# The first batch of a fused attention, mixing and gating kernel: other load queues, other owners for three steps, and four output buffers

## The reference

```python
def _attn_ref(q, k, v):
    B, H, S, D = q.shape
    factor = 4
    ...
    q_d = q.reshape(B, H, Sd, factor, D).mean(axis=3)
    ...
    out_d = sm_attn(q_d, k_d, v_d)
    out_up = np.repeat(out_d, factor, axis=2)
    pos = np.arange(S)
    mask = np.abs(pos[:, None] - pos[None, :]) < factor
    scores = scale * np.matmul(q, k.transpose(0, 1, 3, 2))
    scores = np.where(mask, scores, -1000000000.0)
    ...
    out_local = np.matmul(attn, v)
    return (out_up + out_local).astype(np.float32)

def _moe_ref(x, w_ch1, w_ch2):
    X = np.fft.fft(x, axis=1)
    X = np.fft.fft(X, axis=2)
    mixed = np.real(X).astype(np.float32)
    u = x + mixed
    ...
    un = (u - mu) / np.sqrt(var + 1e-06)
    ch = np.maximum(un @ w_ch1, 0.0) @ w_ch2
    return (u + ch).astype(np.float32)

def _moe2_ref(x, w_val, conv_w, w_out):
    ...
    gate = 1.0 / (1.0 + np.exp(-gate_pre))
    val = x @ w_val
    return (gate * val @ w_out).astype(np.float32)
```

## Time and profile before

| | |
|---|---|
| median of 3 runs | 759.3 us (758.93 to 759.83) |
| the profiled execution | 760.19 us, of which its span 758.3 us |
| TensorE matmul busy | 696.6 us, 92% of the span |
| VectorE, ScalarE, GpSimd busy | 393.0, 186.2, 168.8 us |
| chain that ended last | TensorE 79%, DMA 7%, VectorE 4%, GpSimd 3%, SP's queue 3% |

### The profile page before, as it was taken

The page is one execution under the profiler, slowest core; times in us unless marked ns, Lnnn a source line. Parts: engine busy times, 40 slices in busy tenths (PEclk is TensorE's granted clock), DMA queues, the critical chain, the costliest instruction groups (busy, mean ns, idle before and its releaser), DMA issues.

```text
span 758.3 us, 14783 instructions
## 1 busy us (share of the span) xinstructions
PE 696.6 (92%) x5936; PEld 531.9 (70%) x5936; DVE 393.0 (52%) x937; ACT 186.2 (25%) x405; POOL 168.8 (22%) x155
## 2 busy tenths in 40 slices
PE   2559857999999998999999999999999999999998
PEld 1445445877777776877777877877767877777776
DVE  4437585554644881544845871545754841123451
ACT  1536532222212132322112122221112131111101
POOL 8001477992101221003101321022201200000000
PEclk9999767999999999999999999999999999999999
DMA  9995047213001128025100027034100000000001
GB/s 254 280 243 154 5 169 170 50 50 74 18 2 32 32 63 204 16 57 114 34 1 32 32 69 204 10 78 100 27 1 1 17 24 24 1 1 2 1 24 39
DMA packets 47174, 51.35 MB, mean 68 GB/s; under 512 B 9149, under 2 KB 40192, under 8 KB 46022
## 3 DMA queue, kind: packets, MB, share of 16 engines
q1 hardware_dynamic: 32608, 31.06, 16.4%
q10 hardware_dynamic: 9574, 16.99, 7.2%
q0 software_dynamic: 4928, 2.39, 1.7%
HBM read 43.32 MB, written 4.72 MB: 63 GB/s over the span
## 4 chain that ended last, share of the span: by engine, by line
PE 79%; DMA 7%; DVE 4%; POOL 3%; SPq 3%; issue 2%; ACT 1%; ACTq 0%; POOLq 0%; DVEq 0%
PE Y L597 23%; PE P L580 23%; PE Y L702 4%; PE P L713 4%; PE P L702 4%; DMA kl<-qk_win 3%; PE A L609 3%; PE Y L713 3%; PE A L663 2%; DMA out<-ot 2%; PE A L567 2%; PE A L549 2%; PE A L652 1%; SPq L449 1%; PE A L502 1%
## 5 line engine op out<-in xcount | busy, mean ns | idle before, releaser
L597 PE MATMUL Y<-hT,w 128*128 128x288 f16 x1536 | 214.7, 286 | 0.0
L580 PE MATMUL P<-unT,w_wv 128*128 128x288 f16 x1536 | 210.1, 288 | 4.7 <-DVE hT L1172 3.9
L580 PEld LDWEIGHTS P<-unT,w_wv 128*128 128x128 f16 x1536 | 148.9, 98 | 49.1 <-issue 6.4
L1172 DVE SCALAR_TENSOR_TENSOR hT<-P,hT 128x288 f16<-128x288 f32 x128 | 58.3, 457 | 230.8 <-ACT hT L837 230.5
L597 PEld LDWEIGHTS Y<-hT,w 128*128 128x128 f16 x1536 | 145.9, 98 | 41.8 <-issue 3.5
L837 ACT ACTIVATE hT<-P 128x288 f16<-128x288 f32 x128 | 52.4, 411 | 224.6 <-PE P L580 223.5
L1208 DVE SCALAR_TENSOR_TENSOR gate<-xT,cw,gate 128x288 f32<-128x288 f32 x128 | 66.4, 519 | 4.5
L808 ACT ACTIVATE prob_or_un<-prob_or_un 73x288 f32<-73x288 f32 (+1 forms) x52 | 23.3, 448 | 91.5 <-DVE prob_or_un L1034 87.9
L1362 POOL DMA_DIRECT2D x<-xd x24 | 17.2, 903 | 99.5 <-DVE xd L1062 75.3
L335 POOL TENSOR_TENSOR x<-x,fb 128x256 f32<-128x256 f32 (+1 forms) x12 | 12.0, 1003 | 96.2 <-DVE fb L1113 96.2
L713 PE MATMUL Y<-shared,wo 128*128 128x288 f32 x128 | 32.1, 409 | 0.5 <-DVE shared L1218 0.5
(11 more groups left out here) (169 smaller groups left out, 819.7 us busy)
## 6 DMA issues: line engine op xcount, KB each, us to landing
kl<-qk_win SPq DMA_DIRECT2D x38, 140.0 KB, 7.2
ql<-qk_win SPq DMA_DIRECT2D x19, 256.0 KB, 4.8
vl<-v_win SPq DMA_DIRECT2D x72, 65.0 KB
pair_or_folded<-qk_pool SPq DMA_DIRECT2D x8, 580.0 KB, 5.8
...
```

The source lines that it names most:

```text
L580: last = mm(P[s % 2][:, 0:HN], w1s(k, f, wt), unT[:, ut, k, ha * HN:(ha + 1) * HN], start=k == 0 and wt + ut == 0, stop=k == KD - 1 and wt ...
L597: last = mm(Y[d][:, 0:HN], w2s(f, d, wt), hT[s % 3][:, ht, :], start=f == 0 and wt + ht == 0, stop=f == KF - 1 and wt == 1)
L1172: nc.vector.scalar_tensor_tensor(out=hT[s % 3][:, 1, :], in0=P[s % 2][:, 0:HN], scalar=0.0, in1=hT[s % 3][:, 0, :], op0=ALU.max, op1=ALU.s ...
```

## The change

The arithmetic stays, but for two places in batch 0: the normalisation is computed as x·rstd + shift with shift = −mean·rstd, on ScalarE, and four adds and four pooling instructions are done by another engine.

- Loads. ScalarE no longer issues value windows. SP issues windows of queries and keys 0 and 1, values 0, queries and keys 2, 3, 4, values 4. GpSimd issues values 1 and 2 once queries and keys 1 have landed, and values 3 once queries and keys 2 have (24 instructions in `first_values`). The four loads of w1 are issued at s = 3, 4, 6, 7, those of w2 at s = 12 to 15 (before 7, 8, 11, 12).
- Pooling. In batch 0 one half of the values is pooled by VectorE, in batch 1 both halves (`pool_v` on VectorE, behind the first MLP slice's `hidden_low`). `pool_qk` stands ahead of `unit_norm`.
- Weights. The squares begin at s = 8, the last eight stand behind the last tile copy, and pieces 6 and 7 of w1's high part behind these. `weight_scale(0)` is at s = 13. Both w2 pieces stand behind all of `inv_std`.
- Batch 0's tail. ScalarE normalises (`normalise_first`), VectorE adds u's fourth tile too, transposes of normalised rows 1 and 3 go to the P banks.
- Output. The second half of a batch uses four buffers, the two new ones being `fa` and `fb`, which the folds of the next batch also use. The folds wait for those stores.

```diff
         wtmp = gate[:].rearrange("p d c -> p (d c)").bitcast(f16)[:, 0:2 * WCW].rearrange("p (i c) -> p i c", i=2)
-        ot = [sb(f"ot{i}", [128, HN]) for i in range(2)]
+        ot = [sb(f"ot{i}", [128, HN]) for i in range(2)] + [fa[:, 0:HN], fb[:, 0:HN]]
...
         POOLING_FIRST = {1: 1, 3: 2, 5: 3}
-        WEIGHT_LOADS = {2: [0], 3: [1], 4: [2], 5: [3], 7: [4], 8: [5], 11: [8, 6], 12: [7]}
-        SQUARES = {5: [0, 1], 6: [2, 3], 7: [4, 5], 8: [6, 7], 13: [8], 14: [9, 10], 15: [11], 16: [12, 13]}
-        W1_HIGH = {10: [0, 1], 11: [2, 3], 12: [4], 13: [5], 14: [6], 15: [7]}
-        FIRST_VALUES = {2: (2, 0), 3: (2, 1), 4: (3, 0), 5: (3, 1)}
-        W1_LOW = {11: [0, 1], 12: [2, 3], 13: [4], 14: [5], 15: [6], 16: [7]}
+        WEIGHT_LOADS = {3: [0], 4: [1], 6: [2], 7: [3], 11: [8], 12: [4], 13: [5], 14: [6], 15: [7]}
+        SQUARES = {8: [0], 9: [1, 2], 10: [3, 4], 11: [5, 6], 12: [7]}
+        W1_HIGH = {13: [0, 1], 14: [2, 3], 15: [4, 5]}
+        W1_LOW = {14: [0, 1], 15: [2, 3], 18: [4, 5]}
         SEQ_AT, FEAT_AT = 23, 28
-        W1_AT = 9
+        W1_AT = 13
...
-            if opening(b) and t in (2, 3):
-                return vl_first[t - 2], ld_v_first[t - 2], 1
-            used = t // 2 + 1 if t < 2 else 2
-            return vl[t % 2][:], ld_v[t % 2], used if opening(b) else b * (3 - t % 2) + t // 2
+            if opening(b) and t in (1, 2, 3):
+                return [vl[1][:], *vl_first][t - 1], ld_v_first[t - 1], 1
+            used = 1 if t == 0 else 2
+            return vl[t % 2][:], ld_v[t % 2], used if opening(b) else b * (3 - t % 2) + t // 2 - t % 2
...
-            return (Y[2 * i % 4], Y[(2 * i + 1) % 4]) if opening(b) else (A[i % 2], A[i % 2])
+            return (Y[2 * i % 4], (Y[1], Y[3], P[0], P[1])[i % 4]) if opening(b) else (A[i % 2], A[i % 2])
...
                     window(b, 2, "qk")
-                    window(b, 1, "v")
...
                     if u == 0:
-                        pe.wait_ge(v_pooled, 2 * b + 2)
+                        pe.wait_ge(v_pooled[0], b + 1)
+                        pe.wait_ge(v_pooled[1], b + 1)
...
                         spectrum_part(g, i, bank[g])
-                weight_sum(1)
...
                     spectrum_part(g, 2, bank[g])
+                weight_sum(1)
...
                 pe.wait_ge(un_done, 6 * b + i + 1)
-                if i >= 2:
+                if opening(b):
+                    if i >= 4:
+                        pe.wait_ge(unT_sb, i - 3)
+                elif i >= 2:
                     pe.wait_ge(unT_sb, 6 * b + i - 1)
-                elif not opening(b):
+                else:
...
+            def normalise_first(j):
...
+                act.wait_ge(shift_done, j + 1)
+                for h in range(2):
+                    r = XROWS[j + 3 * h]
+                    if j == 0 and h == 0:
+                        act.wait_ge(transposed, NU)
+                    if j == 2:
+                        act.wait_ge(unT_ps, h + 1)
+                    nc.scalar.activation(un[(2 * j + h) % 4][0:r, :], x[0:r, j + 3 * h, :], ACT.Identity, bias=shift[0:r, j, h:h + 1],
+                                         scale=rstd[0:r, j, h:h + 1]).then_inc(un_done, 1)
...
                     act.wait_ge(out_ps, n + 1)
-                    act.wait_ge(st_out[d % 2], 16 * (4 * b + 2 * ha + d // 2 + 1))
-                    nc.scalar.mul(ot[d % 2][:], (P[d % 2] if ha == 0 else Y[d])[:, 0:HN], 0.5).then_inc(out_sb, 1)
+                    i = d if ha == 1 else d % 2
+                    if i < 2:
+                        act.wait_ge(st_out[i], 16 * (3 * b + (2 if ha == 1 else d // 2) + 1))
+                    nc.scalar.mul(ot[i][:], (P[d % 2] if ha == 0 else Y[d])[:, 0:HN], 0.5).then_inc(out_sb, 1)
                     act.wait_ge(out_sb, n + 1)
-                    act.dma_start(out[b, d * 128:(d + 1) * 128, ha * HN:(ha + 1) * HN], ot[d % 2][:]).then_inc(st_out[d % 2], 16)
+                    act.dma_start(out[b, d * 128:(d + 1) * 128, ha * HN:(ha + 1) * HN], ot[i][:]).then_inc(st_out[i], 16)
...
                     if m is None:
-                        if s in FIRST_VALUES:
-                            first_value_loads(*FIRST_VALUES[s])
...
                 if m is None:
-                    for c in range(WCH + 6, 2 * WCH):
+                    for c in range(WCH, 2 * WCH):
                         weight_square(c)
+                    weight_high(6)
+                    weight_high(7)
...
                         u_columns(b, i, m)
+                        if i % 2 == 0:
+                            normalise_first(i // 2)
...
+            def pool_v(b, k):
...
+                half = raw_values(b, k).rearrange("p (h r) c -> p h r c", h=2)
+                dve.wait_ge(ld_vraw[k], 16 * (b + 1))
+                tt(half[:, 0], half[:, 0], half[:, 1], ALU.add).then_inc(v_half_dve, 1)
+                dve.wait_ge(v_half_dve, 1 if opening(b) else 3 - k)
+                tt(vd[:, k, :, 0:D], half[:, 0, 0].rearrange("p (h c) -> p h c", h=H), half[:, 0, 1].rearrange("p (h c) -> p h c", h=H),
+                   ALU.add).then_inc(v_pooled[k], 1)
...
                         dve.wait_ge(spec, 5 * b)
+                if i == 0 and later(b - 1):
+                    dve.wait_ge(st_out[3], 16 * (b - 1))
+                    dve.sem_inc(passed, 1)
...
                 for s in range(SLOTS if m is not None else S0 + NU + LAG_AV + 4):
+                    if b == 1 and s == 1:
+                        pool_v(b, 1)
+                        pool_v(b, 0)
...
                             unit_shift(b, first + 1)
+                            if s in POOLING_FIRST:
+                                pool_qk(b, POOLING_FIRST[s])
+                            if first == 0:
+                                pool_v(b, 1)
...
                                 unit_scale(b, u)
-                        if s in (POOLING if m is not None else POOLING_FIRST):
-                            pool_qk(b, (POOLING if m is not None else POOLING_FIRST)[s])
+                        if m is not None and s in POOLING:
+                            pool_qk(b, POOLING[s])
...
                 if m is None:
+                    weight_low(6)
+                    weight_low(7)
...
                     combine(b, 0)
+                    add_mixed(tt, 3, ROWS[0], fb, fa).then_inc(u_rev, 1)
...
                     combine(b, 1)
-                    normalise(b, 0)
...
                     combine(b, 2)
-                    normalise(b, 1)
                     columns(b, 0)
+                    columns(b, 1)
                     statistics(b, 2)
-                    columns(b, 1)
-                    normalise(b, 2)
...
                 pool.wait_ge(var_eps, 3 * b + j + 1)
+                if opening(b):
+                    nc.gpsimd.tensor_scalar(shift[0:r, j, :], mv[0:r, j, :, 0], -1.0, None, ALU.mult).then_inc(mean_down, 1)
                 pt(rstd[0:r, j, :], rstd[0:r, j, :], mhalf[0:r, :], ALU.pow).then_inc(rstd_done, 1)
+                if opening(b):
+                    pool.wait_ge(mean_down, j + 1)
+                    pool.wait_ge(rstd_done, j + 1)
+                    pt(shift[0:r, j, :], shift[0:r, j, :], rstd[0:r, j, :], ALU.mult).then_inc(shift_done, 1)
...
             def step(b):
-                if later(b):
+                if later(b) and not (isinstance(b, int) and b == 1):
...
                 zero_rows(b)
+                for j in range(3):
+                    if later(b) or j > 0:
+                        mix_rev(b, j)
+                    inv_std(b, j)
...
                     second_weights(0)
-                for j in range(3):
-                    mix_rev(b, j)
-                    inv_std(b, j)
-                if opening(b):
...
                 pt(half[:, 0], half[:, 0], half[:, 1], ALU.add).then_inc(v_half, 1)
-                pool.wait_ge(v_half, 2 * b + (k if opening(b) else 1 - k) + 1)
+                pool.wait_ge(v_half, 1 if opening(b) else 2 * (b - 2) + (1 - k) + 2)
                 pt(vd[:, k, :, 0:D], half[:, 0, 0].rearrange("p (h c) -> p h c", h=H), half[:, 0, 1].rearrange("p (h c) -> p h c", h=H),
-                   ALU.add).then_inc(v_pooled, 1)
+                   ALU.add).then_inc(v_pooled[k], 1)
...
+            def first_values(t):
...
+                for j in range(2):
+                    for dst, src in value_parts(0, t, j):
+                        pool.dma_start(dst, src).then_inc(values(0, t)[1], 16)
...
             pool_v(0, 0)
-            pool_v(0, 1)
             nc.gpsimd.memset(fdft[0:96, 2, :], 0.0).then_inc(table_zeroed, 1)
-            pool.wait_ge(v_pooled, 2)
+            pool.wait_ge(v_pooled[1], 1)
...
                                   id_sb[0:GQ, 0:GQ].unsqueeze(2).to_broadcast([GQ, GQ, 4])).then_inc(spread_made, 1)
+            pool.wait_ge(zeroed, 7)
+            for t in range(1, 4):
+                _, _, landed, count = keys(0, (0, 1, 1, 2)[t])
+                pool.wait_ge(landed, 48 * count)
```

(2 more changed lines are left out.)

25 lines of the change are left out of this document (15 added, 10 removed).

## The result

| | before | after |
|---|---|---|
| median of the runs, us | 759.1 (6 runs, 757.9 to 765.1) | 747.4 (6 runs, 745.0 to 749.3) |
| ratio, with its 95% interval | | 0.984 (0.981 to 0.987) |
| profiled execution: time, span, us | 760.2, 758.3 | 746.5, 744.7 |
| keys of local tile 1 used | 45.34 | 36.05 |
| first MLP slice of batch 0 | 118.47 | 104.06 |

A forecast was written before the change was run, and what follows sets the result against it. The prediction took the bound to be TensorE nearly throughout behind 120 us, and ahead of it a chain of transfers and engines. Its terms summed to −6.1 us from 759.3, giving 753, with a range of 744 to 759.

The forecast's parts named there:

- keys: Keys of local tile 1, with fewer weight and value loads beside them: usable at 35.5 us in place of 45.34, −9.8.
- to the transposes: From the keys to local tile 0's transposes, 7.64 us before: `weight_scale` leaves this stretch, −0.9.
- to the last copy of transposes: From tile 0's transposes to ScalarE's last copy: same 23.7 us, three tiles at half speed, plus high parts 0 and 1, +0.7.
- to the spectrum copies: From the last copy of transposes, 13.95 us before: ScalarE becomes the bound and needs 18.5, +4.6.
- to the MLP: From the spectrum copies, 27.84 us before: faster VectorE adds and normalisation on ScalarE, less added work and TensorE's restart, −3.3.
- first slices: First to fifth MLP slice, 14.46 us before: VectorE's pooling, held up by GpSimd, delays the second low part, +6.5.
- output buffers and the rest: Third slices of batches 1 and 2: four buffers end TensorE's idle 2.68 and 1.26 us, −3.9.
- The ladder: The five local tiles one behind the other, from tile 0's transposes on; forecast to take the same, apart from +0.7.
- Rival A: VectorE not held up in the first slices, TensorE speeding up early with up to 4 us off slow tiles: 745; chance 0.22.
- rival C: GpSimd's 24 value-load issues become the bound, from 0.95 us an issue; at 1.991 us each the sum is 778; chance 0.10.
- Rival B: The change does not bring the keys forward, 40 us or later: 757.5 to 760, no difference; chance 0.10.

The follow-up runs named there:

- a_pairs_apart: Changed kernel with VectorE's pooling of the keys put back behind the normalisation of the pair before; 0.986 of the time before, span 752.6 us.
- a_squares_behind: Changed kernel with the last four of the eight w2 squares moved behind the spectrum copies; 0.978 of the time before, span 742.1 us.
- a_piece_first: Changed kernel with w2 piece 0 back ahead of the rest of batch 1's mixing on GpSimd; 0.986 of the time before, span 749.2 us.
- a_piece_waits: Changed kernel with GpSimd's w2 piece 1 waiting until VectorE has pooled both raw halves of batch 1; span 740.7 us, one execution.

## Why the prediction was right in sign and short in size

| step | forecast | measured |
|---|---|---|
| keys | −9.8 | −9.3 (45.34 to 36.05) |
| to the transposes | −0.9 | −0.9 (7.64 to 6.73) |
| to the last copy of transposes | +0.7 | −4.4 (23.7 to 19.34) |
| to the spectrum copies | +4.6 | +5.5 (13.95 to 19.5) |
| to the MLP | −3.3 | −5.4 (27.84 to 22.45) |
| first slices | +6.5 | +5.1 (14.46 to 19.55) |
| output buffers and the rest | −3.9 | −4.3 |
| sum | −6.1 | −13.7 (span: −13.6) |

**Keys: right, for a sum that was put wrongly.** 36.05 against 35.5, though with 4.00 us of idle time where I had said under 3. The pairs were quicker than I took them (5.3 us, not 5.9), so TensorE was ready at 32.05, and the transfer decided. I priced a load by the rule that each small packet waits for a large one, 768 turns of 12 ns more: 3.2 us a MB. In the trace 2450 small packets met 466 large ones, not as many. That my price lay near the 2.9 us a MB found above, about the load's own transfer time, was chance. The 1.7 us for the landing in that sum stands in no run.

**The ladder is the term that failed.** "I take the same", three tiles at half speed, was the choice; the rows gave no ground for it but that it had been so. In the profiled execution the first tile's products were already at full rate: from tile 0's transposes to tile 3's it took 12.7 us (42.78 to 55.45), before 17.3 (52.98 to 70.27). Rival A named this, at up to 4 us and a chance of 0.22, and its other half (VectorE not held up) did not happen. Its reason, that TensorE is denser before the tiles, is not shown: a_pairs_apart was to test it and came out otherwise. The experiments make the size softer: in three of the six executions of this code full speed came at 51, and there the same term was −1.6 (a_squares_behind: 42.18 to 64.26).

**Spectrum copies: right in mechanism.** ScalarE became the bound, with the eight squares and two high parts in a row; a_squares_behind shows it, by taking four away. Among the signs I said that ScalarE would have no idle time ahead of them. It had 4.05 us, for low parts that VectorE made between its folds. The sum had the first of these waits (2.99 us), not the second (1.06); that is why 19.5 and not 18.5. TensorE, said to be idle for 3 to 5 us ahead of the feature transform, was idle for 3.31.

**To the MLP: right mechanisms, undersized by 2.1.** VectorE's adds at 0.43 us instead of 1.49, the normalisation off VectorE. a_piece_first prices w2's piece 0 in its old place at 3.2 where I had 2. The cost of TensorE's restart was there too: the 20 matmuls at 83.26 took 4.33 us in place of 2.50, 1.8 where I had 1.2.

**First slices: nearly the right sum, from two parts of which I had one.** I let both halves land 5.8 us after the MLP's start and put a GpSimd instruction ahead of each of VectorE's four. In the trace only the last two were slowed, by 2.2 us (a_piece_waits). The larger part was the second half's transfer, 8.35 us from its issue: it shared the queue with 1.16 MB of batch 1's next keys and queries that were issued right behind it. That this sharing slowed it was not tested; the kernel before issued the same transfers in the same order. There GpSimd waited for them, and TensorE then only 0.50 us for GpSimd.

**Output buffers: right**, alone as in company. **GpSimd's queue** (rival C): an issue took 0.55 to 0.59 us (16 of them in 8.92), far from the 0.95 at which it would have decided:

```profile
41.37 4.47 POOL L1466 DMA_DIRECT2D unT<-v_win  x8
45.83 4.45 POOL L1466 DMA_DIRECT2D xT<-v_win  x8
```

**Rival B** did not occur: the keys came forward. The range held the time, near its lower end: the ladder (5.1 us) and the stretch to the MLP (2.1) came out better than forecast, the other terms within 1.4. That the total stayed in the range owes something to luck, as the ladder alone wanders by 2.8 us.
